# One level of Strassen's scheme in the second MLP's up-projections, and its down-projection in groups of four chunks

## The reference, cut to what matters

```python
x  = attention(q, k, v, mem_k, mem_v)              # 3072 tokens x 512
h  = x @ w_in;  y = (relu(h) + alpha*min(h, 0)) @ w_out     # first MLP, 512 -> 2048 -> 512
a  = y @ w_a;   b = y @ w_b                        # second MLP, 512 -> 1536, twice
out = (a * b) @ w_out2                             # 1536 -> 512
```

## Time and profile before

| | |
|---|---|
| time, median of 3 runs | 1291.52 us (1291.05 to 1291.56) |
| the profiled execution, first to last instruction (the span) | 1288.8 us |
| time around that span, by the median | 2.7 us |
| PE busy | 1259.5 us, 98% |
| PE weight loads (PEld) | 1144.9 us, 89% |
| DVE / ACT / POOL busy | 680.7 / 448.9 / 252.7 us |
| mean granted TensorE clock | 0.991 |

### The profile page before, as it was taken

The page is one execution under the profiler, slowest core; times in us unless marked ns, Lnnn a source line. Parts: engine busy times, 40 slices in busy tenths (PEclk is TensorE's granted clock), DMA queues, the critical chain, the costliest instruction groups (busy, mean ns, idle before and its releaser), DMA issues.

```text
span 1288.8 us, 19051 instructions
## 1 busy us (share of the span) xinstructions
PE 1259.5 (98%) x6800; PEld 1144.9 (89%) x6800; DVE 680.7 (53%) x1246; ACT 448.9 (35%) x1264; POOL 252.7 (20%) x228
## 2 busy tenths in 40 slices
PE   7888999999999999999999999999999999999998
PEld 6788999999999999999999888888888888888887
DVE  7886777777767777777565223322322322322222
ACT  6755555555555555554453101101101100100100
POOL 1676333322233322232010001100100100100000
PEclk9889999999999999999999999999999999999999
DMA  6443211222112122120244100100100100100000
GB/s 254 127 119 113 80 57 56 79 69 83 56 55 79 56 81 70 55 80 19 83 139 132 33 9 25 57 9 1 57 8 0 50 15 0 49 8 0 33 0 33
DMA packets 30088, 74.99 MB, mean 58 GB/s; under 512 B 2912, under 2 KB 7008, under 8 KB 30048
## 3 DMA queue, kind: packets, MB, share of 16 engines
q1 hardware_dynamic: 22896, 62.41, 15.3%
q10 hardware_dynamic: 7152, 12.06, 2.6%
HBM read 61.87 MB, written 12.58 MB: 58 GB/s over the span
## 4 chain that ended last, share of the span: by engine, by line
PE 84%; DVE 8%; ACT 3%; DMA 3%; issue 2%; ACTq 0%; DVEq 0%; SPq 0%
PE bank L443 21%; PE bank L445 21%; PE bank L444 21%; PE bank L637 5%; PE bank L639 5%; PE bank L638 5%; DMA w_raw<-w 2%; PE bank L482 2%; DVE g_hi L986 1%; PE bank L456 1%; DVE g_raw L982 1%; PE bank L455 1%; ACT prob L722 1%; DVE prob L952 1%; PE bank L467 1%
## 5 line engine op out<-in xcount | busy, mean ns | idle before, releaser
L1084 DVE TENSOR_TENSOR p_raw<-a_sb,bank 128x512 f32<-128x512 f32 x72 | 49.5, 688 | 413.5 <-ACT a_sb L873 413.5
L873 ACT ACTIVATE a_sb<-bank 128x512 f32<-128x512 f32 x72 | 43.1, 598 | 505.3 <-PE bank L445 505.3
L982 DVE SCALAR_TENSOR_TENSOR g_raw<-relu_neg,neg_al,g_raw 128x384 f32<-128x384 f32 x128 | 94.6, 739 | 137.7 <-ACT relu_neg L752 137.0
L751 ACT ACTIVATE g_raw<-bank 128x384 f32<-128x384 f32 x128 | 62.6, 489 | 242.4 <-PE bank L445 242.3
L409 POOL TENSOR_TENSOR y_lo<-y_raw,y_hi 128x512 f32 (+1 forms) x24 | 31.7, 1323 | 500.9 <-ACT y_hi L853 500.9
L443 PE MATMUL bank<-y_hi,w_first 128*128 (+1 forms) x264 | 102.8, 389 | 0.0
L445 PE MATMUL bank<-y_hi,w_first 128*128 (+1 forms) x264 | 102.7, 389 | 0.0
L444 PE MATMUL bank<-y_lo,w_first 128*128 (+1 forms) x264 | 102.7, 389 | 0.0
L443 PE MATMUL bank<-y_hi,w_later 128*128 (+1 forms) x264 | 102.7, 389 | 0.0
L444 PE MATMUL bank<-y_lo,w_later 128*128 (+1 forms) x264 | 102.7, 389 | 0.0
L445 PE MATMUL bank<-y_hi,w_later 128*128 (+1 forms) x264 | 102.7, 389 | 0.0
(11 more groups left out here) (130 smaller groups left out, 3219.3 us busy)
## 6 DMA issues: line engine op xcount, KB each, us to landing
u_raw<-units SPq DMA_DIRECT2D x53, 576.0 KB, 3.7
w_raw<-w SPq DMA_DIRECT2D x52, 256.0 KB, 2.7
u_early<-units SPq DMA_DIRECT2D x11, 576.0 KB, 9.3
y_dram<-y_stage ACTq DMA_DIRECT2D x8, 768.0 KB, 3.9
y_raw<-y_dram SPq DMA_DIRECT2D x24, 256.0 KB, 2.7
out<-o_stage ACTq DMA_DIRECT2D x5, 1024.0 KB, 4.4
y_stage<-w SPq DMA_DIRECT2D x16, 256.0 KB, 3.0
out<-o_stage SPq DMA_DIRECT2D x2, 256.0 KB, 2.1
```

The lines of the kernel that those rows point to most:

```text
L751: nc.scalar.activation(g_raw[:, :], h_ps[:, 0:TOK], ACT.Relu)
L873: nc.scalar.activation(a_sb[:, j % 2], a_ps[j % 2][:, :], ACT.Copy).then_inc(a_copied, 1)
L982: nc.vector.scalar_tensor_tensor(out=g_raw[:, :], in0=relu_neg[:, :], scalar=neg_al[:, j:j + 1], in1=g_raw[:, :], op0=ALU.mult, op1=ALU.add)\
L1084: nc.vector.tensor_tensor(p_raw[:, :], a_sb[:, j % 2], b_ps[j % 2][:, :], ALU.mult)\
```

## The change

The second MLP is rewritten. Tokens go in three super-blocks of 1024 (two halves of 512). The 12 chunks go in six pairs. For each pair and each of a and b, the product is a 2x2 block product: the weights are four blocks (chunk of the pair x half of the 512-long sum), y is four blocks (half of the sum x half of the tokens). One level of Strassen's scheme (in the form with seven products and shared sums) replaces the eight block products by seven. Each block product is 2 pieces of the sum by 3 multiplications, so 6 matmuls of 512 columns.

- The sums of y blocks are made once for each super-block, on DVE (`y_sums`), and the seven blocks are split by ACT and POOL (`hi_yc`, `lo_yc`). The sums of weight blocks are made for each pair in each super-block, on POOL (`sum_w1` to `sum_w4`), and split by ACT and POOL (`hi_ws`, `lo_ws`). Weights are no longer kept in SBUF: `load_ab` fetches 1 MB for each of the 18 pairs into one buffer `wr`, and `load_wo` fetches the down-projection's four chunks for each group.
- The seven products go to three pairs of PSUM banks. DVE reads partly accumulated banks between the products (`pair`), and forms the four blocks of a and b and their product a*b.
- The down-projection runs in groups of four chunks (two pairs) for all 1024 tokens: 8 steps (`project`) of 12 matmuls. Group 0 stands behind pair 2 of a super-block, groups 1 and 2 behind pair 5. The result of each group is added in SBUF (`gather`), and stored by SP.
- The stage is unrolled; there are no hardware loops in it. SBUF tensors are laid out by explicit offsets.

The core of the diff. The products come in the order M1, M6, M2, M7, M5, M4, M3; `hi_ws(n + 1, K_M3)` waits for the product M3 of pair n, since the buffer of its weights is the same; `splits_before` gives a group behind pairs 2 and 5 of a super-block; `splits_after` gives the step two further on.

```diff
@@ sync @@
+            def load_y(s, q):
...
+                elif q == 0:
+                    sp.wait_ge(y_stored, 16 * (-(-(s + 1) * TOK2 // TOK)))
+                    sp.wait_ge(p_done, 4 * PAIRS2 * s)
+                else:
+                    sp.wait_ge(yc_lo_done, PRODUCTS * (2 * s + 1))
+            def load_ab(n):
+                if n:
+                    sp.wait_ge(ws_hi_done, PRODUCTS * n)
+                    sp.wait_ge(ws_lo_done, PRODUCTS * n)
...
+            def load_wo(big, c):
+                if 4 * big + c >= 2:
+                    sp.wait_ge(wo_lo_done, 4 * big + c - 1)
...
+            for s in range(SUPERS):
+                for j in range(PAIRS2):
+                    n = s * PAIRS2 + j
+                    if n + 1 < NPAIRS:
+                        load_ab(n + 1)
+                    if n == 1:
+                        for c in range(4):
+                            load_wo(0, c)
+                    for g in {2: (0,), 5: (1, 2)}.get(j, ()):
+                        big = s * GROUPS + g
+                        if g and s + 1 < SUPERS:
+                            load_y(s + 1, g - 1)
+                        if big + 1 < NGROUPS:
+                            for c in range(4):
+                                load_wo(big + 1, c)
+                        if g == GROUPS - 1:
+                            for m in range(SUBS):
+                                store_out(s, m)
@@ gpsimd @@
...
+                    if n + 1 < NPAIRS:
+                        sum_w1(n + 1)
+                        sum_w3(n + 1)
+                        lo_ws(n + 1, K_M1)
+                        sum_w2(n + 1)
+                        lo_ws(n + 1, K_M6)
+                        lo_ws(n + 1, K_M2)
+                        sum_w4(n + 1)
+                        for k in range(K_M7, PRODUCTS):
+                            lo_ws(n + 1, k)
+                    if n == 1:
+                        for c in range(4):
+                            lo_wo(0, c)
+                    for g in {2: (0,), 5: (1, 2)}.get(j, ()):
+                        big = s * GROUPS + g
+                        for m in range(SUBS):
+                            if m % 2 == 0 and big + 1 < NGROUPS:
+                                lo_wo(big + 1, m // 2)
+                            if g and s + 1 < SUPERS:
+                                for q, i in y_splits((g - 1) * SUBS + m):
+                                    lo_yc(s + 1, q, i)
@@ tensor @@
+            def product(n, k, mat):
+                if mat == 0:
+                    pe.wait_ge(ws_lo_done, PRODUCTS * n + k + 1)
+                    if k == 0 and n % PAIRS2 == 0:
+                        pe.wait_ge(yc_lo_done, 2 * PRODUCTS * (n // PAIRS2 + 1))
...
+                elif k == K_M2:
+                    bank_of = x_ps[mat]
+                    pe.wait_ge(m1_copied, 2 * n + mat + 1)
...
+                elif k == K_M4:
+                    bank_of = y_ps[mat]
+                    pe.wait_ge(u3_done, 2 * n + mat + 1)
...
+                for q in range(2):
+                    w = slice((2 * mat + q) * P, (2 * mat + q + 1) * P)
+                    last = add_to(bank_of[:, :], ws[:, k, 0, w], ws[:, k, 1, w], y[:, 0, q], y[:, 1, q],
+                                  q == 0 and k in (K_M1, K_M6, K_M5))
+            def project(big, m):
+                u = big * SUBS + m
+                pe.wait_ge(pl_done, u + 1)
...
+            for s in range(SUPERS):
+                for j in range(PAIRS2):
+                    n = s * PAIRS2 + j
+                    for k in range(PRODUCTS):
+                        product(n, k, 0)
+                        product(n, k, 1)
...
+                    for g in {2: (0,), 5: (1, 2)}.get(j, ()):
+                        for m in range(SUBS):
+                            project(s * GROUPS + g, m)
@@ scalar @@
+            def hi_p(big, m):
...
+                if u >= 2:
+                    act.wait_ge(projected, u - 1)
...
+                    copy_m1(n, 0)
+                    copy_m1(n, 1)
...
+                    if more:
+                        hi_ws(n + 1, K_M1)
+                    if n:
+                        copy_c11(n)
+                    if more:
+                        for k in range(K_M6, K_M3):
+                            hi_ws(n + 1, k)
+                    big = splits_before(n)
+                    if big is not None:
+                        hi_p(big, 0)
+                        hi_p(big, 1)
+                    if more:
+                        hi_ws(n + 1, K_M3)
+                    if n == 1:
+                        for c in range(4):
+                            hi_wo(0, c)
...
+                        for m in range(SUBS):
+                            then = splits_after(big, m)
+                            if then:
+                                hi_p(*then)
+                            if m % 2 == 0 and big + 1 < NGROUPS:
+                                hi_wo(big + 1, m // 2)
+                            if g and s + 1 < SUPERS:
+                                for q, i in y_splits((g - 1) * SUBS + m):
+                                    hi_yc(s + 1, q, i)
@@ vector @@
+            def pair(n):
...
+                for mat in range(2):
+                    m1_plus_y(n, K_M6, mat, u2[:, mat], u2_done)
+                p11 = p_slot(n, 0)[:, 0:HALF2]
+                dve.wait_ge(c11_copied, n + 1)
+                dve.wait_ge(product_done, products(n, K_M2, 1))
+                nc.vector.tensor_tensor(p11, p11, x_ps[1][:, :], ALU.mult).then_inc(p_done, 1)
+                for mat in range(2):
+                    m1_plus_y(n, K_M7, mat, u3[:, mat], u3_done)
...
+                p12 = p_slot(n, 0)[:, HALF2:TOK2]
+                for mat, dst in enumerate((p12, cb[:, 2])):
+                    dve.wait_ge(product_done, products(n, K_M3, mat))
+                    dve.wait_ge(u2_done, 2 * n + mat + 1)
+                    nc.vector.tensor_tensor(dst, z_ps[mat][:, :], u2[:, mat], ALU.add).then_inc(c12_done, 1)
+                dve.wait_ge(c12_done, 2 * n + 2)
+                nc.vector.tensor_tensor(p12, p12, cb[:, 2], ALU.mult).then_inc(p_done, 1)
...
+                    pair(n)
+                    big = splits_before(n)
+                    if big is not None:
+                        lo_p(big, 0)
+                        lo_p(big, 1)
...
+                        for m in range(SUBS):
+                            gather(big, m)
+                            then = splits_after(big, m)
+                            if then:
+                                lo_p(*then)
+                            if g and s + 1 < SUPERS and m in (3, 4):
+                                y_sums(s + 1, g - 1, m - 3)
```

More of the change, by code:

```diff
@@ L40 @@
 CH1, CH2 = FF1 // P, FF2 // P
-TOK2 = 512
-TILES2 = BATCH * SEQ // TOK2
-SUB2 = TOK2 // P
 WU = 512
-W1_UNITS, W2_UNITS = 2 * CH1, 3 * CH2
+W1_UNITS = 2 * CH1
+HALF2 = 512
+TOK2 = 2 * HALF2
+SUPERS = BATCH * SEQ // TOK2
+PAIRS2 = CH2 // 2
+NPAIRS = SUPERS * PAIRS2
+GROUPS = PAIRS2 // 2
+NGROUPS = SUPERS * GROUPS
+SUBS = TOK2 // P
+PRODUCTS = 7
+K_M1, K_M6, K_M2, K_M7, K_M5, K_M4, K_M3 = range(PRODUCTS)
+Y_B11, Y_B21, Y_B22, Y_T1, Y_T3, Y_T2, Y_T4 = range(PRODUCTS)
+USES = {K_M1: Y_B11, K_M6: Y_T2, K_M2: Y_B21, K_M7: Y_T3, K_M5: Y_T1, K_M4: Y_T4, K_M3: Y_B22}
+USED_BY = {block: k for k, block in USES.items()}
+BASE = 16512
 W_STAGE = 2
@@ L645, in tile2 @@
-            def tile2(t2):
-                first = isinstance(t2, int)
-                y_at = 0 if first else pe.snap(parity(t2) * (KT * TOK2))
-                for j in range(CH2):
-                    ab(t2, j, y_at, first)
-                    if j:
-                        project(t2, j - 1, first)
-                    elif first:
-                        down(TILES - 1, CH1 - 1, False)
-                    elif not first:
-                        project(t2 - 1, CH2 - 1, False)
-            tile2(0)
@@ new lines, in _ @@
+            for s in range(SUPERS):
+                for j in range(PAIRS2):
+                    n = s * PAIRS2 + j
+                    for k in range(PRODUCTS):
+                        product(n, k, 0)
+                        product(n, k, 1)
+                        if n == 0 and k == 0:
+                            down(TILES - 1, CH1 - 1, False)
+                    for g in {2: (0,), 5: (1, 2)}.get(j, ()):
+                        for m in range(SUBS):
+                            project(s * GROUPS + g, m)
@@ new lines, in hi_wo, with copy_m1 @@
+            def hi_wo(big, c):
+                act.wait_ge(wo_loaded[c % 2], 16 * (2 * big + c // 2 + 1))
+                if big >= 2:
+                    act.wait_ge(projected, SUBS * (big - 1))
+                else:
+                    act.wait_ge(down_done, TILES * CH1)
+                nc.scalar.activation(wo_slot(big, c)[:, 0], w_raw[:, c % 2], ACT.Copy).then_inc(wo_hi_done, 1)
+            def copy_m1(n, mat):
+                act.wait_ge(product_done, products(n, K_M1, mat))
```

(3 more changed lines are left out.)

630 lines of the change are left out of this document (352 added, 278 removed).

## The result

The changed kernel took **1315.59 us** (median of 4 runs, 1314.32 to 1318.78), the kernel before beside it 1291.47 (4 runs, 1291.05 to 1291.56). The ratio is 1.0187, 95% interval 1.0171 to 1.0203: 24 us slower, where 14.8 had been forecast. The profiled execution of the changed kernel has a span of 1314.5 us, 25.7 more than before. Of the 1.6 us between the two differences, 0.7 is that the profiled run took 1316.25, above the median, and 0.9 that only 1.8 us lie around its span, not the 2.7 that the prediction added.

The account below looks back on a forecast made before the run. TensorE was taken to bound the second MLP alone; 216 matmuls fewer save 49.0 us, against 63.8 us of new idle time and slow clock: +14.8, 1306 us, range 1278 to 1328.

Parts of the forecast that it names:

- The likeliest case, as summed: Whole kernel: new idle time and slow clock outweigh the matmuls saved, 1290 to 1330 us; chance 0.66.
- changes of super-block: Two changes: TensorE waits for the late `wo` load, y's low parts and y sums, 13 us in all (6 to 28).
- group starts: Before six first `project` steps TensorE waits for `lo_p` behind the pair in DVE's queue, 3.6 us each, 21.6 in all.
- the clock: Granted clock falls behind ten idle times of 3 us or more, 1.7 us each, 17 us in all (0 to 34).
- The floor: Least idle time at a group start, for `c12`, p12, `lo_p` and handovers without port waits: 2.4 us.
- Rival B: DVE and POOL's shared port is free at group starts, 2.4 us each: 6.6 us faster, 1285 us; chance 0.21.
- Pair 1 and the `wo` loads: M4 of pair 1 stalls 3.0 us on lagging weights; M2 of pair 2 waits 9.2 us behind first `wo` splits.
- What costs nothing: Satisfied waits, y's split and first weights beside the first MLP's last tile, the end, stores: no delay, 0 us.
- C: POOL becomes the bound, its chain 24.9 us for a pair of 19.0: about 1353 us; chance 0.08.
- D: 252 pieces of 6 matmuls each pay for their own wait, 28 us in all: 1334 us; chance 0.05.

Follow-up runs that it names:

- e5_small_pool: Changed kernel with POOL's weight sums and low parts cut to 8 of 512 columns from pair 1 on (output not the reference's): 1292.36 us in one run.
- e1_lop_early: Changed kernel with each group's first two splits (`hi_p` on ACT, `lo_p` on DVE) moved inside the pair: 1298.46 us, ratio 1.0045 to the kernel before.
- e4_fill_gaps: Changed kernel with eight extra matmuls, their result overwritten, before TensorE's wait at each of six group starts: 1309.54 us, ratio 1.0134 to the kernel before.
- e6_c11_first: Changed kernel with ACT doing `copy_c11(n)` ahead of `hi_ws(n + 1, K_M1)`, which waits for a load: 1317.83 us, ratio 1.0193 to the kernel before.
- e2_wo_later: Changed kernel with `hi_wo(0, 2)` and `(0, 3)` moved from pair 1 to pair 2, behind `copy_c11`: 1316.67 us, ratio 1.0183 to the kernel before.
- e8_reordered_2: e7_reordered with next pair's M4/M3 weight splits behind `hi_p` of steps 0 and 1, and second-half y sums in group 2's steps 0 and 1: 1268.51 us.
- e7_reordered: Changed kernel with all order changes together (group splits, `copy_c11`, `wo` chunks, y's loads, splits and sums), same work: 1283.93 us, ratio 0.9937 to the kernel before.
- e9_pool_in_last_tile: Kernel before, with POOL repeating one y low-part subtraction 14 times in the first MLP's last tile: 1303.98 us, ratio 1.0089 to the kernel before.
- e1 to e6: Six runs, each the changed kernel with one edit: group splits, `wo` splits, super-block change, filler matmuls, less POOL weight work, `copy_c11` order; 1292.36 to 1317.83 us.

## Why the prediction was right, and where it was short

**Direction and mechanism.** The likeliest case, as summed, is what happened: slower, inside the range of 1278 to 1328, by the waits that were named. The measured time lies 9.6 us above the forecast. The changes of super-block (5.8), the later begin (3.7), the small pieces (2.4), the group starts (1.1) and M6 (1.0) are over the forecast, the clock (2.8) is under it.

**Group starts** were 22.7 us for 21.6. The floor was nearly right: 2.4 had been worked out from the end of the last slot, and from there it is 2.27 (the bracket of 2.11 and 0.16; the chain is c12, p12 and `lo_p`, 3 x 0.69). POOL's share was put too low, 1.2 us a start where it is 1.5 as a mean. The place behind the pair costs 2.12 us each time even without POOL's weights (e5_small_pool), operations of 1.7 us instead of 0.69 add the rest, and with another place both are gone (e1_lop_early). The Trainium skill, SBUF — State Buffer, section "SBUF: two separate sides", has a DVE operation with two SBUF inputs and a GpSimd operation that reads SBUF exclude each other for whole instructions. The trace agrees: 1.67 to 1.80 us for 0.69 while POOL is busy, and never over 0.692 with a PSUM input. The pair of numbers that the prediction gave for it, 1.57 for 0.43, is of a cast with one input; the two-input `p_lo` of the earlier trace rows, 0.69 and 1.67, is what bears on it.

**Rival B** held for the last group start alone (2.11). It needed POOL ahead or idle at all of them, and e5_small_pool shows what that would have been worth: 1292.4 us where the kernel before had 1293.1, in one run. Its 1285 put nothing down for y's sums, and their waits of 1.2 and 2.0 us are still there.

**The clock** cost 14.2 us for 17, and e4_fill_gaps shows that it is a cost of its own. Ten falls of 1.7 us behind idle times of 3 us or more had been forecast; there are six such idle times and seven falls. The 3.18 us at 776.39 cost no clock, nor did 2.71 at 737.93, while 2.04 at 1088.55 and 2.11 at 1265.59 did.

**Pair 1 and the `wo` loads** came as worked out, 2.9 for 3.0 and 9.0 for 9.2 (1 MB landed in 4.8 us for 5.1, and POOL's low parts of weights took 1.45 as a mean, over the 1.26 to 1.4 named). What the prediction did not say is that such waits are no independent terms: e6_c11_first and e2_wo_later each removed one and gained nothing, as the wait was passed on to the next step of the same late chain.

**Changes of super-block** were 18.8 for 13. ACT behind the late `wo` load was 2.09 and 0.61 for 2 each, the end of the second half's low parts 0.65 and 0.67 for 2.5 each (the profile names no releaser for these two; POOL's last low part of y ends 0.10 us before each). The mis-sized term is the y sums beside POOL's low parts: 2 us had been put down for both groups, and they cost 1.18 + 2.02 in group 1 and 1.18 + 2.05 in group 2, 6.4. A step has 2.72 us of TensorE, and DVE's work in it rose by two sums of 1.7; e8_reordered_2 shows for group 2 that without POOL beside them they cost nothing.

**The step that failed** is in "What costs nothing": the split of y and the first weights beside the last tile of the first MLP. I asked whether they end in time for pair 0, not what they do to DVE there. DVE makes the y sums there too, and they stand ahead of a `split_g`; beside POOL the five operations take 7.0 us, more than a step of 4.2:

```profile
680.35 1.77 DVE L1249 TENSOR_TENSOR y_sum<-y_in,y_sum 128x512 f32<-128x512 f32 x1
682.16 1.67 DVE L1251 TENSOR_TENSOR y_sum<-y_in,y_sum 128x512 f32<-128x512 f32 x1
683.75 1.65 DVE L1152 SCALAR_TENSOR_TENSOR g_raw<-relu_neg,neg_al,g_raw 128x384 f32<-128x384 f32 x1
685.43 1.30 DVE L1156 CAST g_hi<-g_raw 128x384 fp32r<-128x384 f32 x1
686.77 0.56 DVE L1158 TENSOR_TENSOR g_lo<-g_raw,g_hi 128x384 fp32r<-128x384 f32 x1
```

That is the wait of 2.47 at 687.38. In e7_reordered, where this part of the sums stands one chunk later, it goes with them:

```profile
692.13 0.44 PE L576 MATMUL bank<-g_hi,w_later 128*128 128x384 f32 x1 [2.46 <-DVE g_lo L1166]
```

With the smaller waits TensorE waits 3.3 us for `g_lo`, and the stage begins 3.7 us late. That POOL slows DVE so was shown in the earlier trace rows, and e9_pool_in_last_tile shows it in this place. The 3.7 itself is one profile against one: in the profiles of the runs e1 to e6, whose instructions up to there are those of the changed kernel, the stage begins anywhere from 696.6 to 701.8, with waits for `g_lo` of 3.2 to 3.3 us in all of them. The 1.0 of M6 in pair 1 is the same lag that was priced for M4, one product earlier.

**Rivals C and D** fell. POOL is busy 358 of 613 us, so it is not the bound. A wait that is already satisfied costs nothing that shows: all small pieces together are 2.3 us, where D needed 28.

## What to carry to other kernels

When a change takes work from the bounding engine and gives it to others, its gain is set by each queue's order, not by busy times: the same work gave +1.9% or -1.9%. Where two engines share a port, cost every place in which the moved work runs beside the other engine's due work, the stage before it too, and put it where that engine is idle. Waits along one late chain are not to be removed singly; find what is late at its head, and move all that hangs on it at once.

## What the runs showed of the hardware that was not expected

The length of an idle time alone does not tell whether the clock falls behind it. In the kernel with little POOL work, two group starts have the same 2.12 us. Behind the second the first matmul lasts 0.80 us instead of 0.50, and its window of 10 us is at 0.83:

```profile
765.10 0.50 PE L793 MATMUL bank<-wo,ph 128*128 128x512 f32 x1 [2.12 <-DVE pl L1310]
...
846.40 0.80 PE L793 MATMUL bank<-wo,ph 128*128 128x512 f32 x1 [2.12 <-DVE pl L1310]
```

In the changed kernel 3.18 us (at 776.39) cost no clock, and 3.70 us (at 1181.41) did, window by window:

```profile
770.00:780.00 10.00, 6.82 (x31) 5.28 (x30) 7.16 (x9) 2.76 (x5) 5.57 (x4) 1.00 0.00 0
...
1180.00:1190.00 10.00, 8.59 (x25) 6.82 (x26) 4.42 (x4) 1.15 (x2) 5.47 (x4) 0.66 0.00 0
```

The same group start, with 3.17 us before it, does have a first matmul of 0.80 us in e6_c11_first (at 776.68). What decides it stays open. Also, 1 MB read back from `y_dram` took 6.1 us where 1 MB of packed weights took 4.8, and a POOL operation of 1.29 us alone took 1.72 to 1.74 beside DVE: the delay goes both ways.
